# Mixture-of-experts inputs transposed on TensorE instead of by DMA, in a fused attention and expert kernel

## What is computed

```python
scores = (1/S) * z @ z.T                       # per batch; B=8, S=3072, d_qk=64
x = u * (maximum(scores, 0)**2 @ v)            # D=256, rows of all batches in one list
logits = x @ w_gate                            # E=8 experts
e = argmax(logits); g = softmax(logits)[e]
# row i goes to the next free place of its expert, while that has under 768 rows
h = maximum(disp[e] @ w1[e], 0)                # w1: 8 x 256 x 1024
out[i] = g[i] * (h @ w2[e])[place of i]        # w2: 8 x 1024 x 256; other rows 0
```

## Time and profile before

| | us |
|---|---|
| median of 3 runs | 922.38 |
| lowest, highest | 920.88, 922.82 |
| the profiled execution, its own time | 922.82 |
| its span, first to last instruction | 921.0 |
| TensorE matmuls busy in the span | 878.7 |
| VectorE busy | 633.7 |
| ScalarE busy | 600.2 |
| the expert stage, first hidden matmul to the end of the span (from 658.39) | 262.6 |

### The profile page before, as it was taken

The page is one execution under the profiler, slowest core; times in us unless marked ns, Lnnn a source line. Parts: engine busy times, 40 slices in busy tenths (PEclk is TensorE's granted clock), DMA queues, the critical chain, the costliest instruction groups (busy, mean ns, idle before and its releaser), DMA issues.

```text
span 921.0 us, 22938 instructions
## 1 busy us (share of the span) xinstructions
PE 878.7 (95%) x7503; PEld 696.5 (76%) x7504; DVE 633.7 (69%) x1361; ACT 600.2 (65%) x911; POOL 121.0 (13%) x120
## 2 busy tenths in 40 slices
PE   3999899999999999999999999999699999999995
PEld 1787687788888888888888888888477777777774
DVE  6876667877877988879877877687345564656430
ACT  6877686777877778887887787688244344434421
POOL 0001001101101101101110110110112112121212
PEclk9899999999999999999999999999799999999998
DMA  9954409505504650100100000600624245325100
GB/s 267 211 173 160 159 13 318 199 8 170 171 23 148 192 169 17 34 17 17 34 23 11 34 27 19 184 23 17 122 77 112 69 141 160 91 86 143 51 17 34
DMA packets 110663, 90.78 MB, mean 99 GB/s; under 512 B 46909, under 2 KB 105482, under 8 KB 110640
## 3 DMA queue, kind: packets, MB, share of 16 engines
q1 hardware_dynamic: 105744, 77.84, 29.9%
q0 software_dynamic: 4896, 12.64, 3.8%
HBM read 40.03 MB, written 44.93 MB: 92 GB/s over the span
## 4 chain that ended last, share of the span: by engine, by line
PE 87%; DVE 6%; issue 3%; DMA 2%; ACT 1%; POOLq 1%; POOL 0%; DVEq 0%; SPq 0%
PE Sc L736 14%; PE O L622 14%; PE O L624 14%; PE O L626 14%; PE Sc L600 7%; PE Sc L601 7%; PE O L757 5%; PE O L759 5%; PE O L761 5%; PE M L671 1%; DMA disp<-xrow,slot 1%; PE M L576 1%; DVE attn_hi L887 1%; PE M L654 1%; DMA rawz<-in_z 1%
## 5 line engine op out<-in xcount | busy, mean ns | idle before, releaser
L622 PE MATMUL O<-vS,attn_hi 128*128 128x256 f16 x1332 | 364.8, 274 | 0.7 <-DVE ubuf L937 0.7
L626 PE MATMUL O<-vS,attn_lo 128*128 128x256 f16 x1332 | 364.8, 274 | 0.0
L624 PE MATMUL O<-vS,attn_hi 128*128 128x256 f16 x1332 | 364.8, 274 | 0.0
L430 ACT ACTIVATE Sc<-Sc 128x768 f32<-128x768 f32 x224 | 178.6, 797 | 77.6 <-PE Sc L601 67.6
L893 DVE TENSOR_TENSOR attn_lo<-attn,attn_hi 128x768 f16<-128x768 f32 x224 | 214.7, 958 | 7.7
L434 ACT ACTIVATE attn<-Sc 128x768 f32<-128x768 f32 x224 | 181.5, 810 | 7.1
L600 PE MATMUL Sc<-zP 128*128 (+1 forms) x450 | 147.8, 329 | 7.6 <-ACT attn L434 3.3
L887 DVE CAST attn_hi<-attn 128x768 f16<-128x768 f32 x224 | 125.1, 558 | 41.3 <-ACT attn L434 33.3
L622 PEld LDWEIGHTS O<-vS,attn_hi 128*128 128x128 f16 x1332 | 130.7, 98 | 27.4 <-DVE ubuf L937 1.1
L624 PEld LDWEIGHTS O<-vS,attn_hi 128*128 128x128 f16 x1332 | 130.8, 98 | 26.0 <-issue 0.2
L601 PE MATMUL Sc<-zQ,zP 128*128 (+1 forms) x450 | 147.8, 329 | 0.0
(11 more groups left out here) (137 smaller groups left out, 830.9 us busy)
## 6 DMA issues: line engine op xcount, KB each, us to landing
out<-empty SPq DMA_DIRECT2D x8, 3072.0 KB
wraw<-in_moe_w SPq DMA_DIRECT2D x16, 1024.0 KB, 7.7
rawv<-in_v SPq DMA_DIRECT2D x16, 768.0 KB, 8.2
ubuf<-in_u SPq DMA_DIRECT2D x19, 384.0 KB, 3.2
disp<-empty SPq DMA_DIRECT2D x8, 774.0 KB, 16.8
rawz<-in_z SPq DMA_DIRECT2D x3, 768.0 KB, 6.1
disp<-xrow,slot POOLq DMA_INDIRECT x54, 3.1
rawz<-in_z SPq DMA_DIRECT2D x2, 384.0 KB, 4.5
```

The lines of the kernel that those rows point to most:

```text
L430: act.activation(pair, pair, ACT.Relu).then_inc(s["relu_done"], 1)
L622: nc.tensor.matmul(o_part(t), hi, v[:, 0:D], start=c == 0 and j == 0 and t % 2 == 0, stop=False, skip_group_check=True)
L624: nc.tensor.matmul(o_part(t), hi, v[:, D:2 * D], start=False, stop=False, skip_group_check=True)
L626: ins = nc.tensor.matmul(o_part(t), lo, v[:, 0:D], start=False, stop=c == PAIRS - 1 and j == 1, skip_group_check=True)
```

## The change

The transposing DMA and the small one beside it are replaced by one plain DMA, which brings whole rows of 258 words into `xg` (again over `vS`), rows on partitions. The transposition is done on TensorE: `x_transposes`, 12 transposes of 128x128 float16 values, six of the high half into the PSUM bank `Mh[0]` and six of the low half into `Mh[1]`. ScalarE copies the high half to `xh` (`x_hi`), VectorE the low half to `xl` (`x_lo`), both over the space of `rawv` and two deep. The transposes of group j + 1 stand ahead of hidden 2 of group j; the copies stand behind the relu and the subtraction of part 2 of group j; the first group's are done ahead of the loop. Part 0 of `hidden` waits for both copies instead of for the load. The factors and row numbers are read from `xg`.

```diff
+        xg = vS[:, :, :].rearrange("p c d -> p (c d)").bitcast(F32)[:, 0:4 * TILES * XW].rearrange(
             "p (b t d) -> p b t d", b=4, t=TILES)
...
-            def load_rows(at, k):
-                sp.dma_start_transpose(xt[:, k, :, :], disp_halves[bass.ds(at, GROUP), 0:2 * D]
-                                       ).then_inc(s[f"loaded_x{k}"], 16)
-                sp.dma_start(tail[:, k, :, :], disp[bass.ds(at, GROUP), D:D + 2].rearrange("(t p) d -> p t d", p=P)
-                             ).then_inc(s[f"loaded_t{k}"], 16)
...
             for k in range(4):
-                load_rows(k * GROUP, k)
+                sp.dma_start(xg[:, k, :, :], disp[k * GROUP:(k + 1) * GROUP, :].rearrange("(t p) d -> p t d", p=P)
+                             ).then_inc(s[f"loaded_x{k}"], 16)
...
+            def x_hi(j, half):
+                act.wait_ge(s["xT2_psum"], 2 * j + 1)
+                act.activation(xh[:, half, :, :].rearrange("p m n -> p (m n)"), Mh[0], ACT.Copy
+                               ).then_inc(s["xh_ready"], 1)
...
+            x_hi(0, 0)
             high(0, 0)
             high(1, 1)
...
+                        if p == 0:
+                            only_if(act, True if k < 3 else i < E // 2 - 1, lambda: x_hi(j + 1, (k + 1) % 2))
...
+            def x_transposes(i, k):
+                pe.wait_ge(s[f"loaded_x{k}"], i * 16 + 16)
+                for h in range(2):
+                    for m in range(DC):
+                        for t in range(TILES):
+                            at = h * D + m * P
+                            ins = nc.tensor.transpose(Mh[h][:, m * GROUP + t * P:m * GROUP + (t + 1) * P],
+                                                      xg_halves[:, k, t, at:at + P], identh[:, :])
+                    ins.then_inc(s["xT2_psum"], 1)
+            x_transposes(0, 0)
...
                 if p == 0:
-                    pe.wait_ge(s[f"loaded_x{k}"], i * 16 + 16)
+                    pe.wait_ge(s["xh_ready"], j + 1)
+                    pe.wait_ge(s["xl_ready"], j + 1)
...
                 for k in range(4):
+                    only_if(pe, True if k < 3 else i < E // 2 - 1, lambda: x_transposes(*((i, k + 1) if k < 3 else (i + 1, 0))))
                     hidden(i, k, 2)
...
+            def x_lo(j, half):
+                dve.wait_ge(s["xT2_psum"], 2 * j + 2)
+                dve.tensor_copy(xl[:, half, :, :].rearrange("p m n -> p (m n)"), Mh[1]).then_inc(s["xl_ready"], 1)
...
+            x_lo(0, 0)
             row_factors(0, 0)
             row_factors(0, 1)
             low(0, 0)
...
+                        if p == 0:
+                            only_if(dve, True if k < 3 else last, lambda: x_lo(j + 1, (k + 1) % 2))
```

More of the change, by code:

```diff
@@ L145, in relu2_attention_moe @@
         fac = sb("fac", [P, 4, TILES], F32)
-        over_s = vS[:, :, :].rearrange("p c d -> p (c d)")
-        xt = over_s[:, 0:4 * 2 * DC * GROUP].rearrange("p (b m n) -> p b m n", b=4, m=2 * DC)
-        tail = over_s.bitcast(F32)[:, 4 * DC * GROUP:4 * DC * GROUP + 4 * TILES * 2].rearrange(
+        xg = vS[:, :, :].rearrange("p c d -> p (c d)").bitcast(F32)[:, 0:4 * TILES * XW].rearrange(
             "p (b t d) -> p b t d", b=4, t=TILES)
-        disp_halves = disp.bitcast(F16)
+        xg_halves = vS[:, :, :].rearrange("p c d -> p (c d)")[:, 0:8 * TILES * XW].rearrange(
+            "p (b t d) -> p b t d", b=4, t=TILES)
         over_v = rawv[:, :, :].rearrange("p c d -> p (c d)").bitcast(F16)
-        hh, hl = (over_v[:, 8 * q * GROUP:(8 * q + 8) * GROUP].rearrange(
+        xh, xl = (over_v[:, q * 2 * DC * GROUP:(q + 1) * 2 * DC * GROUP].rearrange(
+            "p (b m n) -> p b m n", b=2, m=DC) for q in range(2))
+        hh, hl = (over_v[:, (4 * DC + 8 * q) * GROUP:(4 * DC + 8 * q + 8) * GROUP].rearrange(
             "p (b j n) -> p b j n", b=4, j=2) for q in range(2))
-        w1l = [w1l0[:, :, :], over_v[:, 16 * GROUP:16 * GROUP + DC * F].rearrange(
+        w1l = [w1l0[:, :, :], over_v[:, (4 * DC + 16) * GROUP:(4 * DC + 16) * GROUP + DC * F].rearrange(
             "p (m f) -> p m f", m=DC)]
@@ L188, in relu2_attention_moe @@
             wpart_ready wmax_ready wallmax_ready wscale_ready whi_ready wlo_ready w_step
-            loaded_x0 loaded_x1 loaded_x2 loaded_x3 loaded_t0 loaded_t1 loaded_t2 loaded_t3
+            loaded_x0 loaded_x1 loaded_x2 loaded_x3 xT2_psum xh_ready xl_ready
             h_ready hh_done hl_done y_summed y_ready y_scattered0 y_scattered1 y_scattered2
@@ L328, in _ @@
                     wait_apart(sp, s[f"y_scattered{k}"], i * 48 + 48)
-                    load_rows((j + 4) * GROUP, k)
+                    sp.dma_start(xg[:, k, :, :], disp[bass.ds((j + 4) * GROUP, GROUP), :]
+                                 .rearrange("(t p) d -> p t d", p=P)).then_inc(s[f"loaded_x{k}"], 16)
         @block.gpsimd
@@ L387, in _ @@
                             out=out, out_offset=bass.IndirectOffsetOnAxis(
-                                ap=tail[:, k, t, 1:2].bitcast(U32), axis=0),
+                                ap=xg[:, k, t, D + 1:D + 2].bitcast(U32), axis=0),
                             in_=ybuf[:, k % 2, t, :], in_offset=None, bounds_check=B * S - 1, oob_is_err=False,
@@ L723, in hidden @@
                 q = j * HPAIRS + p
-                par = k // 2
+                par, half = k // 2, k % 2
                 if p == 0:
-                    pe.wait_ge(s[f"loaded_x{k}"], i * 16 + 16)
+                    pe.wait_ge(s["xh_ready"], j + 1)
+                    pe.wait_ge(s["xl_ready"], j + 1)
                     pe.wait_ge(s["wlo_ready"], (i * 2 + par) * 4 + 2)
@@ L731, in hidden @@
                     pe.wait_ge(s["hl_done"], q - 1)
-                terms = [(w, x, m) for w, x in ((w1h, 0), (w1h, DC), (w1l, 0)) for m in range(DC)]
+                terms = [(w, x, m) for w, x in ((w1h, xh), (w1h, xl), (w1l, xh)) for m in range(DC)]
                 for fi in range(2):
@@ L736, in hidden @@
                         ins = nc.tensor.matmul(Sp[:, 2 * (p % 2) + fi, 0:GROUP], w[par][:, m, f * P:(f + 1) * P],
-                                               xt[:, k, x + m, :], start=(at == 0), stop=(at == len(terms) - 1))
+                                               x[:, half, m, :], start=(at == 0), stop=(at == len(terms) - 1))
                 ins.then_inc(s["h_ready"], 1)
@@ L1179, in row_factors @@
             def row_factors(i, k):
-                dve.wait_ge(s[f"loaded_t{k}"], i * 16 + 16)
-                dve.tensor_scalar(fac[:, k, :], tail[:, k, :, 0:1].rearrange("p t a -> p (t a)"),
+                dve.wait_ge(s[f"loaded_x{k}"], i * 16 + 16)
+                dve.tensor_scalar(fac[:, k, :], xg[:, k, :, D:D + 1].rearrange("p t a -> p (t a)"),
                                   winvp[:, k // 2:k // 2 + 1], None, ALU.mult).then_inc(s["fac_ready"], 1)
+            def x_lo(j, half):
+                dve.wait_ge(s["xT2_psum"], 2 * j + 2)
+                dve.tensor_copy(xl[:, half, :, :].rearrange("p m n -> p (m n)"), Mh[1]).then_inc(s["xl_ready"], 1)
             def low(q, p):
```

## The result

The changed kernel takes 934.25 us (median of 4 runs, 933.46 to 936.75), the kernel before 922.43 (920.88 to 922.82). The ratio is 1.013 with a 95% interval of 1.0108 to 1.0150: slower by 10 to 14 us. The profiled execution of the changed kernel took 933.74 us, its span is 932.0.

The account below looks back on a forecast made before the run. TensorE, busy 200.00 of 200.00 us in the expert loop, was taken as the bound. 10.05 us in the loop plus 2.1 at the start gave 12.15, forecast 934.5 us (62%), range 931.5 to 937.0 (90%).

Parts of the forecast that it names:

- The bundle: Expert loop, TensorE: 12 transposes a group cost 0.67 us, all on the path, 15 times: 10.05 us (up to 12.15).
- L671's 0.81: Existing 12-transpose bundle taking 0.81 us; 0.14 read as waiting for VectorE's rows. Rival: switching cost, 2.1 us more, 8%.
- The copies: Expert loop: 0.81 us on ScalarE and 0.56 on VectorE a group fit into holes, cost 0; late-copy rival 942.0, 4%.
- The loads and their move: Expert loop: removing transposing and tail DMAs gains 0; rows wanted 7.83 us sooner cost 0, with 19 us to spare.
- The start: Seam before the expert loop: transposes, VectorE's copy and 0.05 us delay the first hidden matmul by 2.1 us.
- The clock: Seam: transposes do not bring TensorE's clock back, so all 2.1 us stay; an early return would leave +1.1.
- The drain: Seam: POOL's drain ends last, at 658.10, releasing the first transpose; rival that transposing DMAs lengthen it: -1.5 us, 20%.
- My mark for being wrong: Signs against the forecast: TensorE idle in the loop, its first work before 657.5, or a bundle over 0.75 us.

Follow-up runs that it names:

- e1: Kernel before with only the 15 bundles of 12 TensorE transposes added in the loop, their output unread: 931.21 us against 922.17.
- e2: Kernel before with only the 15 copies on ScalarE and on VectorE added in the loop, into unused space: 922.08 us against 922.17.
- e3: Kernel before with only the loads changed to plain DMAs, hidden matmuls reading untransposed rows: 921.45 us against 922.17.
- e4b: Changed kernel with the first group still through a transposing DMA, its tile's copies ahead of the first relu and first subtraction: 932.42 us against 922.04 for the kernel before.
- e7: Kernel before with 134 unused transposes on TensorE while it waits at the seam: 919.92 us against 922.04.
- e11: Changed kernel with 72 more transposes at its start, ahead of the first bundle: 936.09 us (one run), against 921.78 for the kernel before.
- e4: Changed kernel with the first group still through a transposing DMA, ScalarE's copy of its tile behind the second relu: 933.62 us against 922.17 for the kernel before.
- e5: Changed kernel without POOL's drain at the seam: 936.65 us against 921.78 for the kernel before, ratio 1.0152 to 1.0178.

## Why the prediction was right

Forecast 934.5, measured 934.25; 12.15 us by the sum, 12.7 by the two traces from the drain's end, 11.8 by the medians. The terms held one by one, so the range was no luck. That the two medians agree to 0.25 us is: the medians of before alone moved by 1.7 us between the sets of runs.

- *The bundle.* Forecast 0.67 us and 15 of them; measured 0.67 and a period of 16.33. The reading of L671's 0.81 as a wait for its rows was right: in the loop no bundle waited. 56 ns a transpose came about in e1 and in the changed kernel. The 81 ns that the Trainium skill (TensorE: Matmul & The Clock Gate, "Back-to-back issue gap") has for such a stream didn't.
- *The copies.* Forecast free, with 4.6 to 5 us from the start of part 2 to their end and some 3 us to spare. From the start of the hidden matmuls at 715.01 it was 4.4 us, and 3.4 us were left. e2 shows that they crowd nothing.
- *The loads and their move.* Forecast 0; e3 measures nothing that can be told from 0. No bundle in the loop waits for a load.
- *The start.* Forecast 2.1 us from the transposes to the copy's end; measured 2.06, and e4b, which leaves it out, is 2.7 shorter from the drain's end, the difference in the clock included. One detail was off: ScalarE's copy, not VectorE's, is named as the releaser, though it ended at 658.2 and VectorE's at 658.6, 0.1 us before the first hidden matmul. By the ends it was VectorE's, as forecast.
- *The clock.* The number held (I took nothing beyond the 2.1; the two traces have +0.5, within what executions differ) and its reason was wrong, which is luck. I took from the earlier trace rows that transposes don't bring the clock back. e7 and e11 show that they hold it and raise it: 7.6 us at full speed, and the rise 3.8 us after the first. The Trainium skill (TensorE: Matmul & The Clock Gate, "PE-mode transpose") has them not count for the clock; where it and these two runs differ, the runs decide. What kept the clock low after the first bundle is then not the kind of the work. The bundle is short (1.44 us) and is followed by 0.77 us of idling; in the earlier trace rows it is the same, with 1.12 us. In the six traces that start with hidden matmuls at the low clock and have no such gap, the rise came 3.8 us (e1), 4.2 (e3), 4.5 (before, e4b), 4.9 (e4) and 5.0 (e2) after the first of them. In the two with the bundle and the gap it came 7.8 (after) and 6.2 (e5) after the first transpose, and 5.5 and 4.0 after the first hidden matmul, about as if the bundle had not been there. That the gap is what undoes it fits all of these; no run changed the gap alone, so it isn't shown.
- *The drain.* It ended last, as forecast, and kept its length. My mark for being wrong, a first work before 657.5, was badly chosen: TensorE started at 656.51, because attention had ended earlier in that execution. It should have been counted from the drain.

The forecast rested on the loop being full of TensorE's work, and that held: the two engines that got the copies had room, and the DMA engines that were relieved were not waited for.

## What to carry to other kernels

On a stretch where one engine is busy 100%, moving work to it costs its full price however small the instructions, and relieving the DMA engines gives nothing; a bundle of the same kind elsewhere in the kernel is the price list, if the waits inside it are taken off first. Where that engine stands idle at a seam between stages, look at its clock on the far side: cheap idle work through the wait, matmuls or transposes, gave back about 2 to 3 us here (2.8 by the medians, 1.9 by the traces, 3.2 and 3.4 in the changed kernel). A step that ends last at a seam can be a debt and not a wait: with the drain taken out, the end of the program grew by 4.4 us, and with the drain behind the signal neither the seam nor the end paid for it.

## What the hardware showed that I had not expected

- Transposes on TensorE kept its clock up and raised it: 134 back to back kept it at 1.00 for 7.6 us, and 72 at the low clock brought it from 0.50 to 1.00 after 3.8 us.
- POOL's drain lasts 4.476 us in every trace that has it, whatever SP is doing beside it, and if it is left out the program ends 4.4 us later after the last scatter. What it is that POOL still has to do then, I didn't find out.
- The drain and the first transposing load end within a microsecond of each other at the seam of the kernel before: in e7 the load was the later one. The chain of waits names only one of them.
- The clock came back 3.8 to 5.0 us after the first hidden matmul in five traces with the seam of the kernel before or, for that part, the same one (before, e1 to e4). Half of such a spread, 0.6 us, is what a time read from a single pair of traces can be off by at this seam.
